# When VectorE takes a pair's reciprocals, and in which order it parts, subtracts and masks

## What is computed

```python
# attention: q, k, v (4, 8, 576, 64), causal window of 64 keys
scores = scale * np.matmul(q, k.transpose(0, 1, 3, 2))
scores = np.where((rel >= 0) & (rel < 64), scores, -1e9)
attn = np.exp(scores - scores.max(-1)); attn /= attn.sum(-1) + 1e-9
x = heads side by side of (attn @ v)               # (2304, 512)
# a gated product without activation
x = ((x @ w1) * (x @ w2)) @ w3 @ w_out             # 512 -> 1024 -> 512
# 8 experts, the best one for each row
e = argmax(x @ w_gate); out = p[e] * sigmoid(x @ w_output_gate)[e] * (relu(x @ ew1[e]) @ ew2[e])
```

## Time and profile before

| | |
|---|---|
| median of 3 runs | 744.53 us (743.5 to 746.02) |
| the profiled execution | 746.4 us, of which the span from first to last instruction is 744.6 us |
| PE busy | 711.2 us, 96% of the span |
| DVE busy | 374.4 us, 50% |
| ACT busy | 267.0 us, 36% |
| POOL busy | 121.6 us, 16% |
| mean granted PE clock | 0.979 of full speed |

### The profile page before, as it was taken

The page is one execution under the profiler, slowest core; times in us unless marked ns, Lnnn a source line. Parts: engine busy times, 40 slices in busy tenths (PEclk is TensorE's granted clock), DMA queues, the critical chain, the costliest instruction groups (busy, mean ns, idle before and its releaser), DMA issues.

```text
span 744.6 us, 15001 instructions
## 1 busy us (share of the span) xinstructions
PE 711.2 (96%) x5075; PEld 647.7 (87%) x5076; DVE 374.4 (50%) x711; ACT 267.0 (36%) x651; POOL 121.6 (16%) x179
## 2 busy tenths in 40 slices
PE   8986799899999989989999999999999999999997
PEld 7976799799999978989999999878888888888886
DVE  4667756742226754665221348856365654562211
ACT  4442533222114322431220225535264644462222
POOL 7213400010001001000000000212122222121211
PEclk9999799999999989998999999999999999999999
DMA  9865112140012133201600004474447572601010
GB/s 331 266 222 166 37 42 58 44 148 15 1 43 65 37 99 99 62 28 32 255 5 16 29 14 170 141 256 156 143 168 232 192 232 77 230 33 53 27 50 29
DMA packets 44590, 80.12 MB, mean 108 GB/s; under 512 B 4413, under 2 KB 24893, under 8 KB 44544
## 3 DMA queue, kind: packets, MB, share of 16 engines
q1 hardware_dynamic: 39504, 64.01, 26.3%
q0 software_dynamic: 5040, 15.47, 6.0%
HBM read 70.03 MB, written 10.49 MB: 108 GB/s over the span
## 4 chain that ended last, share of the span: by engine, by line
PE 75%; DVE 14%; ACT 7%; issue 3%; DMA 1%; POOLq 0%; DVEq 0%; POOL 0%; ACTq 0%
PE bank L484 22%; PE bank L486 21%; PE bank L485 21%; DVE pT L1027 5%; ACT prob L818 4%; PE bank L759 2%; DVE sm L1011 2%; PE bank L600 2%; DVE prob L1015 1%; PE bank L575 1%; DVE ab_f L1140 1%; PE bank L737 1%; ACT abh L892 1%; DVE nmx L1017 1%; DMA xs<-x_rows,gidc 1%
## 5 line engine op out<-in xcount | busy, mean ns | idle before, releaser
L484 PE MATMUL bank<-Wh,abh 128*128 128x272 f32 (+1 forms) x288 | 85.0, 295 | 9.8 <-DVE abl L1142 9.8
L818 ACT ACTIVATE prob<-prob,nmx 128x64 f32<-128x64 f32 x144 | 48.2, 336 | 105.7 <-DVE nmx L1017 105.7
L486 PE MATMUL bank<-Wh,abl 128*128 128x272 f32 (+1 forms) x288 | 82.5, 287 | 0.0
L485 PE MATMUL bank<-Wl,abh 128*128 128x272 f32 (+1 forms) x288 | 82.5, 286 | 0.0
L1118 DVE TENSOR_TENSOR wbuf<-raw,wbuf 128x1024 f32 (+1 forms) x64 | 75.4, 1222 | 12.5 <-ACT wbuf L884 12.4
L1319 DVE TENSOR_TENSOR hTl<-bank,hTh 128x512 fp32r<-128x512 f32 x44 | 28.4, 686 | 97.9 <-ACT hTh L934 97.9
L484 PE MATMUL bank<-wbuf,hTh 128*128 (+1 forms) x176 | 70.7, 402 | 0.6 <-issue 0.6
L484 PE MATMUL bank<-wbuf,xsTh 128*128 (+1 forms) x176 | 70.5, 400 | 0.0
L486 PE MATMUL bank<-wbuf,hTl 128*128 (+1 forms) x176 | 68.8, 391 | 0.0
L485 PE MATMUL bank<-wbuf,xsTh 128*128 (+1 forms) x176 | 68.7, 390 | 0.0
L486 PE MATMUL bank<-wbuf,xsTl 128*128 (+1 forms) x176 | 68.6, 390 | 0.0
(11 more groups left out here) (218 smaller groups left out, 1471.1 us busy)
## 6 DMA issues: line engine op xcount, KB each, us to landing
raw<-in_expert_w SPq DMA_DIRECT2D x64, 512.0 KB, 4.4
qT<-in_qT SPq DMA_DIRECT2D x24, 192.0 KB, 3.2
kT<-in_kT SPq DMA_DIRECT2D x24, 192.0 KB, 3.6
x_rows<-x_sb POOLq DMA_DIRECT2D x18, 256.0 KB, 2.3
w3r<-in_w3T SPq DMA_DIRECT2D x8, 512.0 KB, 5.5
wo<-in_w_out SPq DMA_DIRECT2D x8, 256.0 KB, 7.9
woT<-in_w_outT SPq DMA_DIRECT2D x4, 512.0 KB, 8.3
vA<-in_v SPq DMA_DIRECT2D x16, 128.0 KB, 2.1
```

The costliest lines, as they stand in the source:

```text
L484: pe.matmul(dst, lh, rh, start=first, stop=False)
L485: pe.matmul(dst, lh, rl, start=False, stop=False)
L486: return pe.matmul(dst, ll, rh, start=False, stop=last)
L818: ex_i = act.activation(pr, pr, ACT.Exp, bias=nmx[:, c:c + 1], accum_out=sums[:, c:c + 1])
```

## The change

Two things are moved; no instruction is added or removed.

First, `weigh` of a pair is done one step later, two steps behind its scores where it was one. In the chunks pair 0 goes from step 0 to step 1, and pair p > 0 from step 2p - 1 to step 2p. In the fold pair 1 goes from i = 4 to 5, and the pairs 2 to 5 from i = 5, 7, 9, 11 to 6, 8, 10, 12. POOL's `normal` is moved in its order with it. Second, `value_lo` stands ahead of `masks` at the end of a step, where it stood behind.

```diff
         def weighed(e):
-            return 0 if e == 0 else (e + 1) // 2 if e % 2 and (e + 1) // 2 < NP else None
+            return 0 if e == 1 else e // 2 if e >= 2 and e % 2 == 0 and e // 2 < NP else None
...
         def fold_weighed(i):
-            return i - 3 if i in (3, 4) else weighed(i - 2) if i > 4 else None
+            return {3: 0, 5: 1}.get(i, i // 2 - 1 if i >= 6 and i % 2 == 0 and i // 2 - 1 < NP else None)
...
+                if i >= 2 and valued(i - 2) is not None:
+                    value_lo(0, valued(i - 2), 0)
                 if fold_scored(i) is not None:
                     masks(0, fold_scored(i))
-                if i >= 2 and valued(i - 2) is not None:
-                    value_lo(0, valued(i - 2), 0)
...
+                    if b is not None and valued(e) is not None:
+                        value_lo(b, valued(e), parity)
                     if b is not None and scored(e) is not None:
                         masks(b, scored(e))
-                    if b is not None and valued(e) is not None:
-                        value_lo(b, valued(e), parity)
```

## The result

The changed kernel takes 750.62 us (median of 6 runs, 749.68 to 752.49) against 743.47 us (6 runs, 741.53 to 746.02): a ratio of 1.0097 with a 95% interval from 1.0074 to 1.0119. It is slower by 7.15 us, where 7.2 was forecast.

A forecast was written before the change was run, and what follows sets the result against it. DVE-ACT circles, not PE, were taken to bound the fold and the stretch before each chunk's first row tile. Fold 2.4 plus three chunks 4.8 made 7.2 us: 744.53 + 7.2 = 751.7 us, range 747.5 to 757.0.

The forecast's parts named there:

- the two circles of DVE and ACT: Fold: a DVE-ACT chain of 11.8 us a turn sets the pace; chunks: one leads to PE's 3.26 us wait for abl.
- The wait is renamed: DVE's 44.3 us of waits for exponentials become waits for a_sb and Wh, which ACT makes behind the same exponentials.
- small gain of 0.06 us a step: Chunk steps 3, 5 and 7: DVE freed of the reciprocals gains 0.06 us each (0 to 0.10).
- The prices: DVE pays 0.31 us for reciprocals (0 to 0.45) and 0.47 for value_lo ahead of masks (0.4 to 0.6).
- 0.23 less 0.06: Chunk step 2: reciprocals cost only 0.23 of 0.31 us, ab_f being held by PE's product; step 3 gains 0.06.
- The chunk: Each of three chunks: last abl 1.6 us later (0.6 to 2.4), PE's wait 3.26 to 4.9 us; +4.8 in all.
- The fold: Fold: value_lo 3 x 0.47 and reciprocals 3 x 0.31, 2.3 us up to the last exponentials; +2.4 at its end (1.2 to 3.2).
- reciprocals of the last pair absorbed without cost: Fold, pair 5: the reciprocals' 0.31 us on DVE vanish, since its piece of w1 waits for POOL anyway.
- Rival C: Fold: POOL's piece of w1 gets ahead of w3l of i = 12, DVE loses 2.4 us; 754.1 us; chance 0.10.
- A: Chunks and fold: the wait for exponentials was a real bound, so PE gains 9.8 and 6.8 us; 728 us; chance 0.05.
- B: Fold: PE's release by value_lo decides, -6.8 us, chunks +4.8; 742.5 us; chance 0.10 together with a no-change variant at 744.5.
- D: The clock rival; 755.6 us; chance 0.07.

The follow-up runs named there:

- fourth experiment: Changed kernel, but in the chunks ACT makes exponentials behind the next tile's a_sb and abh, with reciprocals three steps behind the scores; 733.58 us, ratio 0.9841.
- fifth experiment: As the fourth experiment, and in the fold too exponentials one half product later, reciprocals three half products behind the masks; 717.81 us, ratio 0.9654.
- ninth experiment: Changed kernel with ACT alone altered, in fold and chunks: exponentials one step later, behind the high parts; 714.61 us, ratio 0.9597.
- eighth experiment: Changed kernel, but in the fold the last pair's reciprocals stay at i = 11 as before; 752.40 us, run once.
- third experiment: Kernel before with both moves in the fold alone, chunks as before; 746.51 us, ratio 1.0032.
- first experiment: Kernel before with only the reciprocals moved, in fold and chunks; value_lo stays behind the masks; 746.73 us, ratio 1.0030.
- 10: As the fifth experiment, but value_lo behind the masks again, in fold and chunks; 718.76 us, ratio 0.9657.
- sixth experiment: Kernel before, fold untouched and value_lo behind masks, with the fourth experiment's ACT order and reciprocals in the chunks; 731.25 us, ratio 0.9830.

## Why the prediction was right

**What bounds.** Right: the two circles of DVE and ACT, in the fold and ahead of the row tiles. The fourth experiment cut the one in the chunks and gained 17 us on the changed kernel, the fifth cut the one in the fold as well and gained another 15.8, with nothing else altered but the reciprocals' place. The ninth altered ACT's order alone and gained 36. One link of the fold's circle was missing in the forecast, though: GpSimd. `w3l` ends only 1.08 us behind GpSimd's low part of w2, as these two lines of the changed kernel show, while in the ninth experiment, where no GpSimd instruction runs beside it, it takes 1.22 us (third line):

```profile
67.02 2.35 POOL L1453 TENSOR_TENSOR w2l<-w2r,w2h 128x1024 fp32r<-128x1024 f32 x1 [7.82 <-ACT w2h L835]
68.27 2.18 DVE L1048 TENSOR_TENSOR w3l<-w3r,w3h 128x1024 fp32r<-128x1024 f32 x1 [0.57 <-ACT w3h L829]
...
55.97 1.22 DVE L1050 TENSOR_TENSOR w3l<-w3r,w3h 128x1024 fp32r<-128x1024 f32 x1
```

In the kernel before it is the same, GpSimd from 65.22 for 2.41 us and `w3l` from 66.46 for 2.24. So about 1 us of every turn belongs to GpSimd, before and after alike, and the forecast of a difference isn't touched by it. The chain of the earlier trace rows gives `w3l` 0.24 us and doesn't name GpSimd. No run took this microsecond out by itself.

**The wait is renamed.** Right: of 44.3 us of waits for exponentials 2.8 are left, and 38.2 for `a_sb` and 11.9 more for `Wh` have come. The small gain of 0.06 us a step that was summed for it did not come: from the start of `nmx` to `ab_f` it is 3.17 us before (116.17 to 119.34) and after (118.45 to 121.62).

**The prices.** 0.31 us for the reciprocals and 0.47 for `value_lo`, as measured in the chunks of the trace after. For the step in which the reciprocals' cost and the small gain from the freed odd steps meet, 0.23 less 0.06, or 0.17 us, was summed: `ab_f` to `ab_f` around step 3 of chunk 0 took 10.82 us before and 121.62 - 110.59 = 11.03 after, 0.21 more.

**The chunk.** 1.6 forecast, 1.70 measured; the wait 4.9 forecast and 4.92 measured.

**The fold.** 2.4 forecast, 2.2 measured up to the last values; but that the two are so close is luck, since two errors cancel. The sum had 2.3 us up to `w3l` of i = 12. In fact this `w3l` starts 51.19 us behind the mark (80.74 in the trace after) and started 49.51 behind it, 1.7 later. The three turns from `w3l` to `w3l` are 0.74, 0.72 and 0.66 us longer where 0.78 each had been summed, and ahead of them DVE gained 0.44, which no term had: its gap in front of the first of these `w3l` went from 1.01 to 0.57 us, and no run shows why. In the kernel before the first and the last of these `w3l` are the first two lines; the third is the first one in the changed kernel:

```profile
43.88 1.23 DVE L1048 TENSOR_TENSOR w3l<-w3r,w3h 128x1024 fp32r<-128x1024 f32 x1 [1.01 <-ACT w3h L829]
78.27 2.23 DVE L1048 TENSOR_TENSOR w3l<-w3r,w3h 128x1024 fp32r<-128x1024 f32 x1 [0.58 <-ACT w3h L829]
...
44.23 1.23 DVE L1048 TENSOR_TENSOR w3l<-w3r,w3h 128x1024 fp32r<-128x1024 f32 x1 [0.57 <-ACT w3h L829]
```

The other 0.5 us arise behind that `w3l`, at the last pair, for which the sum had nothing. The eighth experiment, in which the last pair's reciprocals stay where they were, confirms the split: its F is 1.6 us above before. Of the 2.2 us a part comes back behind the fold, G being 0.9 us shorter, so chunk 0 starts only 1.3 later.

**A misread.** The forecast had the reciprocals of the last pair absorbed without cost, and DVE's piece of w1 waiting out GpSimd as before. In fact the sums waited 2.35 us there and the piece of w1 not at all (1.21). Rival C had the right cause, GpSimd's piece directly behind its piece of w2, but named `w3l` or the piece of w1 as the instruction that would be kept waiting, for one more piece, 2.4 us; `w3l` kept its length (2.23 before, 2.18 after). The misread was worth only 0.5 to 0.6 us, since one wait took the other's place: 0.64 us is what the eighth experiment got back.

**The other rivals.** A and B needed a gain from the waits for exponentials or for `xTl`; both waits shrank, by 41.5 and 8.5 us, and nothing came of it. D, the clock, is neither confirmed nor ruled out. In the two traces after waits of 4.9 instead of 3.3 us the stretches from the end of the wait to the next chunk are 24.65, 24.94 and 23.46 us, against 23.53, 25.43 and 24.51, in sum 0.4 less, not 3.9 more. But the third experiment, with the same waits of 3.25 us as before, has 23.52, 22.91 and 23.52, in sum 3.5 less than before. So one trace of each kernel can't show an effect of this size. Over the executions, the mean granted clock was 0.978 to 0.988 in the 29 of the kernel before that stand beside the first experiments, and those at 0.982 and above took 740.8 to 744.8 us, the others 744.95 to 747.0; in the six of the changed kernel it was 0.978 to 0.981. Some of the 7.15 us may therefore be the clock's.

**The whole.** 2.2 in F, -0.9 in G and 3 x 1.7 - 0.4 in the chunks make 6.0 us; the two profiled spans differ by 750.7 - 744.6 = 6.1, and the medians by 7.15. The forecast's own terms, F and C, make 2.2 + 3 x 1.7 = 7.3 against 7.2; what G and the stretches behind the waits take off again in this pair of traces was not forecast. So the mechanism and the size of both terms are right, and the agreement to the tenth of a us is luck.

## What to carry to other kernels

Before moving an instruction out of a wait, look what the next instruction on that engine will wait for: if both are released by the same work of another engine, the wait keeps its end and the moved instruction loses its cover. A small instruction is free inside a wait of the circle that bounds and costs its full issue time outside. When a traced instruction takes twice as long as its like elsewhere (`w3l`, 2.2 against 1.2 us), look what runs beside it on GpSimd before you count it as work. If an engine's long step stands ahead of a short one that others need, move that long step: here the two moves on DVE cost 7 us alone, and ACT's exponentials put one tile (in the fold, one half product) later brought the same kernel to 30 us below the one before.

## What the runs showed of the hardware

An instruction of VectorE on 128 x 6 elements with a single operand, the sum with 1e-9, took 2.35 us beside GpSimd's subtraction of two operands in SBUF (the low part of w1), where it takes 0.17 elsewhere; it ended at 85.19 us and GpSimd's instruction at 85.17. The same stands in other traces, as of the experiments 1, 3, 5 and 10 (2.37, 2.35, 1.47 and 1.46 us). GpSimd's piece took 3.37 us there, since it had itself come while `w3l` was running, and 2.37 next to it. VectorE's `turn_out`, with one operand in a bank, ran beside that next piece at its usual 2.27 us. The Trainium skill, SBUF — State Buffer, section "SBUF: two separate sides", says that a VectorE instruction in a 2-port mode takes the lock as well as one with two operands in SBUF. The trace agrees in the wait; in which mode the sum ran no row shows. The small size of the instruction did not spare it the wait.

`w3l` and `normal` are a pair of the same kind. In the fifth experiment the reciprocals stand ahead of `w3l` and release GpSimd's `normal`, which takes 0.83 us, and `w3l` takes 1.76; in the ninth they stand behind it and `w3l` takes 1.22. The circle of the fold is 8.55 us in the one and 8.15 in the other.

The cost of a wait of PE isn't its length alone. The same work of PE from the last values of the fold to chunk 0 (G) took 6.15, 5.22 and 3.75 us after waits of 4.07, 2.34 and 1.07 us, in the kernel before, the changed one and the first experiment. In the rows of these stretches (columns as in the earlier trace rows) the third number from the end is the granted clock, 0.55, 0.67 and 1.00 of full speed; the lower of its two levels (1.2 of 2.4 GHz) is 0.50:

```profile
90.22:96.37 6.15, 6.15 (x63) 5.61 (x64) 2.12 (x3) 0.89 (x2) 0.00 (x0) 0.55 0.26 67
...
93.23:98.45 5.22, 5.22 (x63) 4.73 (x63) 2.03 (x3) 0.89 (x2) 0.00 (x0) 0.67 0.30 78
...
90.73:94.48 3.75, 3.75 (x64) 3.36 (x64) 1.97 (x3) 0.89 (x2) 0.00 (x0) 1.00 0.35 102
```

The other traces agree: after waits of 2.34 to 2.52 us G is 5.11 to 5.25 in six kernels, after 1.07 to 1.89 it is 3.74 or 3.75 in four, and after 4.10, in the sixth experiment, 5.74. In the kernel before the clock fell while PE stood still, in the changed one about 1 us after the wait had ended. So with one move alone chunk 0 starts 66.1 and 66.5 us behind the mark, earlier than the 67.6 of before, although the values come 0.93 and 1.25 us later. This was seen at one place of the program only. At another the length of the wait did not decide: after the wait for `abl` in chunk 2, 3.26 us before and 3.25 in the third experiment, the same work took 25.43 us at a mean granted clock of 0.89 and 22.91 us at 1.00.
